# q and k loaded in 48 rows a group, and the first chunks' gates, exponents and low parts of w_in in another order

## The reference

```python
m_new = np.maximum(f_gate[:, :, t] + m, i_gate[:, :, t])
f_stab = np.exp(f_gate[:, :, t] + m - m_new)
i_stab = np.exp(i_gate[:, :, t] - m_new)
C = f_stab[..., None, None] * C + i_stab[..., None, None] * np.einsum('bhd,bhe->bhde', vt, kt)
n = f_stab[..., None] * n + i_stab[..., None] * kt
denom = np.maximum(np.abs(np.einsum('bhd,bhd->bh', n, qt)[:, :, None]), 1.0)
y[:, :, t] = sigmoid(o_gate[:, :, t]) * np.einsum('bhde,bhe->bhd', C, qt) / denom
```

## Time and profile before

| | us |
|---|---|
| median of 3 runs | 278.72 |
| lowest and highest | 278.70, 279.81 |
| the profiled execution's own time | 278.94 |
| its span | 277.1 |

### The profile page before, as it was taken

One profiled execution on the slowest core, in us unless ns is written; L12 is line 12 of the kernel. 1 busy time (PEld: TensorE's weight loads), 2 busy tenths in 40 slices (PEclk: granted clock), 3 DMA queues, 4 the chain that ended last, 5 costly groups with the idle time before them and its releaser, 6 DMA issues.

```text
span 277.1 us, 5247 instructions
## 1 busy us (share of the span) xinstructions
PE 269.2 (97%) x1959; PEld 257.6 (93%) x1959; DVE 202.4 (73%) x367; ACT 165.7 (60%) x329; POOL 69.0 (25%) x101
## 2 busy tenths in 40 slices
PE   8889999999999999999999999999999999999995
PEld 6777989889999999999999999999999999999995
DVE  5687987787988988655467686456867776876694
ACT  7968877996886664323243212256576567666763
POOL 6484532166454322063000790000000000000000
PEclk9999999999999999999999999999999999999999
DMA  6789975465546000009400000000000000300004
GB/s 176 227 229 285 296 231 196 143 207 160 184 117 228 2 0 2 0 0 269 151 0 2 0 0 2 0 0 0 4 0 2 0 0 2 142 0 4 0 0 146
DMA packets 13258, 23.61 MB, mean 85 GB/s; under 512 B 1968, under 2 KB 7920, under 8 KB 13232
## 3 DMA queue, kind: packets, MB, share of 16 engines
q1 hardware_dynamic: 12832, 22.89, 27.1%
q10 hardware_dynamic: 400, 0.38, 0.4%
HBM read 21.25 MB, written 2.02 MB: 84 GB/s over the span
## 4 chain that ended last, share of the span: by engine, by line
PE 83%; DVE 7%; ACT 6%; issue 2%; DMA 1%; SPq 0%; DVEq 0%; ACTq 0%
PE bank L592 18%; PE bank L649 14%; PE bank L634 14%; PE bank L617 8%; PE bank L578 7%; PE bank L559 7%; PE bank L536 6%; PE bank L506 3%; PE bank L514 2%; PE bank L542 1%; DMA og_b<-og 1%; PE bank L525 1%; DVE win_lo L988 1%; ACT decay L751 1%; DVE decay L983 1%
## 5 line engine op out<-in xcount | busy, mean ns | idle before, releaser
L592 PE MATMUL bank<-wsp_hi,vn_hi 128*128 128x384 f32 x96 | 32.2, 335 | 0.0
L592 PE MATMUL bank<-wsp_lo,vn_hi 128*128 128x384 f32 x96 | 32.1, 334 | 0.0
L592 PE MATMUL bank<-wsp_hi,vn_lo 128*128 128x384 f32 x96 | 32.1, 334 | 0.0
L796 ACT ACTIVATE gt_hi<-gated_t 128x384 fp32r<-128x384 f32 x16 | 8.4, 524 | 37.1 <-DVE gated_t L1117 37.1
L649 PE MATMUL bank<-wo_hi,hg_hi 128*128 128x320 f32 x96 | 29.8, 311 | 0.3 <-DVE hg_lo L1167 0.3
L649 PE MATMUL bank<-wo_lo,hg_hi 128*128 128x320 f32 x96 | 29.6, 308 | 0.0
L649 PE MATMUL bank<-wo_hi,hg_lo 128*128 128x320 f32 x96 | 29.6, 308 | 0.0
L1150 DVE SCALAR_TENSOR_TENSOR tap<-h,conv_w,tap 128x768 f32<-128x768 f32 (+1 forms) x17 | 16.5, 970 | 17.5 <-ACT tap L828 17.5
L751 ACT ACTIVATE decay<-log_in,cols 128x128 f32<-128x128 f32 x80 | 25.5, 391 | 4.1 <-PE bank L536 4.0
L536 PEld LDWEIGHTS bank<-v_aug,decay 128*128 128x128 f32 x192 | 24.0, 191 | 2.6 <-DVE decay L983 1.3
L834 ACT ACTIVATE gate<-convd 128x768 f32<-128x768 f32 (+1 forms) x17 | 13.8, 809 | 19.3 <-DVE convd L1154 19.3
(11 more groups left out here) (171 smaller groups left out, 766.7 us busy)
## 6 DMA issues: line engine op xcount, KB each, us to landing
qk<-qk SPq DMA_DIRECT2D x24, 160.0 KB
log_in<-neg_m SPq DMA_DIRECT2D x10, 256.0 KB, 5.0
wsp_raw<-w_sp SPq DMA_DIRECT2D x6, 384.0 KB, 3.9
win_raw<-w_in SPq DMA_DIRECT2D x4, 512.0 KB, 5.6
v_aug<-v SPq DMA_DIRECT2D x12, 168.0 KB, 4.4
kw<-k SPq DMA_DIRECT2D x10, 160.0 KB, 4.9
out<-y SPq DMA_DIRECT2D x10, 160.0 KB, 1.9
og_b<-og SPq DMA_DIRECT2D x3, 480.0 KB, 9.9
```

The source lines that it names most:

```text
L592: op = pe.matmul(p_mix[m % 2][:, 0:NB], vs[:, b * NC + c, ds_], ws[:, c, ts], start=(i == 0), stop=(i == len(terms) - 1))
```

## The change

Seven things are altered, all of them before about chunk 3 except the first, which holds for every chunk.

1. q and k come in pieces of 48 rows a group in place of 40. The array in DRAM has the eight further rows, which hold zeros.
2. On SP, one load of og is left ahead of q and k (chunk 0's); og of chunks 1 and 2 is one load behind chunk 1's v. v of chunk 0 goes ahead of the second piece of chunk 0's q and k.
3. On ACT only chunk 0's gates are opened first. Chunks 1 and 2 are opened together in step n = 1, behind `xt_high(0)`, with a change of table to Sigmoid and one back. The memset of `win5_lo` goes from ACT to DVE.
4. On ACT both groups' exponents of chunk 0 come ahead of the gates' exponents (`gate_g`, `gate_w`), and `pad_log(2)` behind these. On DVE `weigh(0, 0)` comes ahead of `gate_diag`. On PE `first_logs(1, 0)` comes ahead of `columns()`.
5. The v half of w_in is split by its two blocks of 128 rows: ACT makes two high parts, DVE makes the first low part ahead of `combine(0)` and the second behind `xt_low(0)`. In every `hidden_v` the product with the second low part is the last one, and in chunk 0 it has a wait of its own.
6. `narrow_copy` of the v half goes behind the exponents of chunk 1.
7. `to_state(2)` moves from the end of step 1 into step 2, behind `in_chunk(2, 0)`, and `new_state(2)` on DVE behind `weigh(2, 1)`.

```diff
@@ SP
-            for g, ps in enumerate((rows(0), rows(1))):
+            for g in range(G):
                 if n == 0 and g:
                     load_k(0)
+                    load_v(0)
                     sp.wait_ge(sem("pad0_high"), 1)
-                sp.dma_start(qk_in[n % RING][ps, :, :, :].rearrange("p a j t -> p (a j t)"), qk[n, ps, :]
+                sp.dma_start(qk_in[n % RING][g * LO:g * LO + QR, :, :, :].rearrange("p a j t -> p (a j t)"),
+                             qk[n, g * QR:(g + 1) * QR, :]
                              ).then_inc(sem(f"ld_qk{n % RING}"), 16)
...
-        for c in range(3):
-            sp.dma_start(og_b0[:, c, :], og[:, c, :]).then_inc(sem(f"ld_og{c}"), 16)
+        sp.dma_start(og_b0[:, 0, :], og[:, 0, :]).then_inc(sem("ld_og"), 16)
         load_qk(0)
         load_in(v_half, "v")
-        load_v(0)
...
         load_v(1)
+        sp.dma_start(og_b0[:, 1:3, :], og[:, 1:3, :]).then_inc(sem("ld_o0a"), 16)
@@ PE, hidden_v
+            last = products.pop()
+            products += [(xt5[p][:, cs], win5_hi[:, fs]), (xt5[p][:, cs], win5_lo[:, fs]), last]
             for i, (lhs, rhs) in enumerate(products):
+                if n == 0 and i == len(products) - 1:
+                    pe.wait_ge(sem("win_low"), 2)
@@ PE, the order
         scores(0)
-        columns()
         pe.wait_ge(sem("neg_ready"), 1)
         first_logs(1, 0)
+        columns()
...
             in_chunk(n, 0)
+            if n == 2:
+                to_state(n)
             hidden_v(n - 1)
...
-            if gives_state(n + 1):
+            if gives_state(n + 1) and n > 1:
                 to_state(n + 1)
@@ ACT
-        for c in range(3):
-            act.wait_ge(sem(f"ld_og{c}"), 16)
-            act.activation(o_gate(c), o_gate(c), ACT.Sigmoid).then_inc(sem("o_ready"), 1)
-            if c == 0:
-                pad_log(2)
+        open_gates(0)
...
         exp_log(0, 0)
+        exp_log(0, 1)
         act.wait_ge(sem("logs_ready"), 2)
         act.activation(sc["g"][:, :], sc["glog"][:, :], ACT.Exp).then_inc(sem("gw_ready"), 1)
         act.activation(sc["w"][:, :], sc["wlog"][:, :], ACT.Exp).then_inc(sem("gw_ready"), 1)
-        exp_log(0, 1)
-        act.activation(win5_lo[LO:128, :].rearrange("p (x t) -> p x t", x=8),
-                       ident[LO:128, :].unsqueeze(1).to_broadcast([LO, 8, 128]), ACT.Copy, scale=0.0).then_inc(sem("win_ready"), 1)
+        pad_log(2)
         narrow_high("v", v_half)
-        win_high("v", v_half)
-        pad_log(0)
+        for t in range(2):
+            win_high("v", v_half, slice(t, t + 1))
         exp_log(1, 0)
-        narrow_copy("v", v_half)
+        pad_log(0)
...
             if n == 1:
+                narrow_copy("v", v_half)
                 xt_high(0)
+                open_gates(1)
@@ DVE
         dve.tensor_copy(cols[:, 2, :], p_cols[:, 2, 0:R]).then_inc(sem("cols_ready"), 1)
+        dve.memset(win5_lo[LO:128, :].bitcast(F32), 0.0).then_inc(sem("win_ready"), 1)
...
+        weigh(0, 0)
         dve.wait_ge(sem("gw_ready"), 1)
         dve.tensor_scalar(diag_dec[:, :], ident[0:R, 0:R], sc["g"][:, L - 1:L], None, ALU.mult
                           ).then_inc(sem("diag_ready"), 1)
-        weigh(0, 0)
         weigh(0, 1)
...
-        first_low(0, v_half)
+        first_low(0, v_half, slice(0, 1))
...
             weigh(n, 0)
-            if n == 2:
-                new_state(n)
             xt_low(n - 1)
+            if n == 1:
+                first_low(1, v_half, slice(1, 2))
...
             weigh(n, 1)
-            if n == 1:
+            if n in (1, 2):
                 new_state(n)
```

More of the change, by code:

```diff
@@ L22 @@
 KS = LO + D
+QR = 48
 EARLY = 2
@@ L549, in hidden_v @@
                 pe.wait_ge(sem("win_ready"), 1)
-                pe.wait_ge(sem("win_hi"), 3)
+                pe.wait_ge(sem("win_hi"), 4)
                 pe.wait_ge(sem("win5_low"), 1)
@@ L565, in hidden_u @@
             if gr == 0 and pair == 0:
-                pe.wait_ge(sem("win_hi"), 6)
+                pe.wait_ge(sem("win_hi"), 7)
                 pe.wait_ge(sem("win5_low"), 2)
-                pe.wait_ge(sem("win_low"), 2)
+                pe.wait_ge(sem("win_low"), 3)
                 pe.wait_ge(sem("exp_done"), 2 * EARLY)
@@ L715, in open_gates @@
         def open_gates(i):
-            act.wait_ge(sem(("", "ld_o0b", "ld_o1", "ld_o1")[i]), (0, 16, 32, 32)[i])
-            piece = og_b0[:, 3:6, :] if i == 1 else og_b1[i - 2][:, :, :]
+            act.wait_ge(sem(("ld_og", "ld_o0a", "ld_o0b", "ld_o1", "ld_o1")[i]), (16, 16, 16, 32, 32)[i])
+            piece = (og_b0[:, 0:1, :], og_b0[:, 1:3, :], og_b0[:, 3:6, :], og_b1[0], og_b1[1])[i][:, :, :]
             act.activation(piece, piece, ACT.Sigmoid).then_inc(sem("o_ready"), 1)
@@ L850, in write_y, with win_high @@
                     act.dma_start(out[b, c * L:(c + 1) * L, :], y[:, c, :]).then_inc(sem("stored"), 16)
-        def win_high(half, cs):
+        def win_high(half, cs, ts):
             act.wait_ge(sem(f"ld_win{half}"), 16)
-            act.activation(win_hi[:, :, cs], win_raw[:, :, cs], ACT.Copy).then_inc(sem("win_hi"), 1)
+            act.activation(win_hi[:, ts, cs], win_raw[:, ts, cs], ACT.Copy).then_inc(sem("win_hi"), 1)
         def narrow_high(half, cs):
@@ L860, in narrow_copy @@
         def narrow_copy(half, cs):
-            act.wait_ge(sem("win_hi"), 1 if half == "v" else 5)
+            act.wait_ge(sem("win_hi"), 1 if half == "v" else 6)
             act.activation(win5_hi[LO:128, cs], win5_hi[0:K5, cs].bitcast(F32), ACT.Copy).then_inc(sem("win_hi"), 1)
         exp_log(0, 0)
+        exp_log(0, 1)
         act.wait_ge(sem("logs_ready"), 2)
@@ L892, in scalar_program @@
             if n == 2:
-                open_gates(1)
+                open_gates(2)
             if n > 2:
@@ L898, in scalar_program @@
             if n == LATE:
-                open_gates(2)
                 open_gates(3)
+                open_gates(4)
             if n + 1 < NS:
@@ L984, in weigh, with first_low @@
                               ).then_inc(sem("weights_ready"), 1)
-        def first_low(i, cs):
-            dve.wait_ge(sem("win_hi"), (2, 4)[i])
-            dve.tensor_tensor(win_lo[:, :, cs], win_raw[:, :, cs], win_hi[:, :, cs].bitcast(F32), ALU.subtract
+        def first_low(i, cs, ts):
+            dve.wait_ge(sem("win_hi"), (2, 3, 5)[i])
+            dve.tensor_tensor(win_lo[:, ts, cs], win_raw[:, ts, cs], win_hi[:, ts, cs].bitcast(F32), ALU.subtract
                               ).then_inc(sem("win_low"), 1)
@@ L1075, in combine @@
             dve.wait_ge(sem("ratio_done"), n + 1)
-            if n < 3 or n % 3 == 0:
-                dve.wait_ge(sem("o_ready"), n + 1 if n < 3 else n // 3 + 3)
+            if n == 1 or n % 3 == 0:
+                dve.wait_ge(sem("o_ready"), n // 3 + 2 if n else 1)
             wait(dve, sem("xt_raw"), n)
@@ L1303, in paired @@
         a = a.reshape(B, J, G, NC, L, D).transpose(0, 3, 2, 5, 1, 4).reshape(NS, G, D, J * L)
-        t = np.zeros((NS, KS, J * L), np.float32)
-        t[:, 0:D], t[:, LO:KS] = a[:, 0], a[:, 1]
+        t = np.zeros((NS, G * QR, J * L), np.float32)
+        t[:, 0:D], t[:, QR:QR + D] = a[:, 0], a[:, 1]
         return t
```

9 lines of the change are left out of this document (4 added, 5 removed).

## The result

The changed kernel is slower: 280.86 us (median of 18 executions, 279.47 to 281.57) against 279.06 (18 executions) for the kernel before, a ratio of 1.0049, 95% [1.0032, 1.0066]. The forecast was 278.3 us and no change that can be told; the time lies outside the forecast's range as well. In all that follows, an execution over 1.5% above the fastest of its kernel counts in the medians, but not in the ratios. The profiled execution of after took 281.11 us, its span 279.3, so 2.2 us more than before.

A forecast was written before the change was run, and what follows sets the result against it. PE, busy 269.2 of 277.1 us, was taken as the bound, with DVE and ACT nearly full too at 25 to 35 us; 0.45 us gained from 278.94 gave 278.5, a median of 278.3, range 277.1 to 279.4.

The forecast's parts named there:

- The sum: Whole kernel: lead at x(0) 1.6, less 0.9 on ACT, less 0.66 on DVE, plus 0.4 of the stall: 0.45 us gained.
- The bound: PE busy 269.2 of 277.1 us; the end moves by what the start of `in_chunk(3, 0)`, 35.23, moves.
- Scores of chunk 0 at 8.1: Head: q and k land for PE's first scores at 8.1 in place of 8.68 us, floor 7.95.
- the 8% of bytes: Loads up to chunk 0's scores: 88 of 1056 KB less, worth 0.4 to 0.7 us if only bytes count.
- T = 16.45: End of `xt_high(0)` on ACT: 16.45 in place of 18.04, 1.6 us earlier; bounds 15.9 and 17.0.
- ACT carries 9.15 us: ACT from the end of `xt_high(0)` to that of `xt_high(1)`: 9.15 us back to back, with two table loads and a Sigmoid.
- So `xt_high(1)` ends ... of 1.6 us of lead 0.7 is left.: ACT in step 1: `xt_high(1)` ends at 25.6, DVE's `xt_low(1)` starts 25.65 instead of 26.36.
- Rival B: ACT's pair of table loads in step 1 becomes the bound and the kernel is slower: middle 279.4 us, chance 0.14.
- Rival D: The skill page's drain holds at ACT's table switches: 2.8 us more on ACT, 281.0 us, chance 0.02.
- `new_state(2)` ahead of `win_lo`, 0.66: DVE: `new_state(2)` now stands between `weigh(2, 1)` and `win_lo`, costing 0.66 us of lead.
- The stall of `shift`, 0.4: DVE at 32.77: `shift` took 1.10 us beside POOL's mask; an earlier mask gains 0.4 us, bounds 0.95 gained, 0.7 lost.
- The other chunks' 48 rows add 64 KB each to queues that have room after 35 us ..., and PE waits for none of them.: DMA queues of later chunks: 0.63 busy after 35 us, so the added rows cost nothing.

The follow-up runs named there:

- e1: The changed kernel again, word for word: 280.98 us, ratio 1.0048 to the kernel before.
- e7: The changed kernel with the gates of chunks 3 to 5 opened one step later (n = 3): 280.38 us, ratio 1.0048.
- e11: The changed kernel with 40 rows and `to_state(2)`, `new_state(2)` where they stood before: 280.89 us, ratio 1.0058.
- e8: The kernel before with only the new order of the head (parts 4, 5, 6, memset on DVE), 40 rows, three gates first: 279.01 us, ratio 0.9989.
- e12: e8 with two matmuls of no use in PE's gap of 0.51 us ahead of `hidden_v(1)`: 279.10 us, ratio 1.0002.
- e3: The kernel before with q and k loaded in 48 rows a group, nothing else: 280.70 us, ratio 1.0038.
- e14: e8 with one single-element Sigmoid behind `xt_high(0)`, which brings two table loads in step 1: 279.30 us, ratio 0.9995.
- e9: e8 with `to_state(2)` and `new_state(2)` moved as in the change: 279.05 us, ratio 0.9992.
- e5: The kernel before again, word for word: 279.04 us, ratio 0.9987.
- e10: e8 with q and k in 48 rows a group as the only other edit: 280.31 us, ratio 1.0032.
- e2: The changed kernel with q and k loaded in 40 rows a group again: 280.46 us, ratio 1.0054.
- e4: The changed kernel with the gates of chunks 0 to 2 loaded and opened first again: 283.22 us, ratio 1.0104.
- e6: The changed kernel with three matmuls of no use in PE's gap ahead of `hidden_v(1)`: 280.32 us, ratio 1.0043.
- e13: e11 with four matmuls of no use in PE's gap ahead of `hidden_v(1)`: 279.77 us, ratio 1.0020.

## Why the prediction was wrong, point by point

The sum gave a gain of 0.45 us where 1.8 us were lost. Two of its steps failed: ACT's lateness was priced only as a later start of DVE's chain, and the other chunks' 48 rows were put at nothing. The rest of the list says what each term measured.

- **The bound.** Right: PE is busy almost throughout, and the stretch to 35 us decides. After it the kernel runs nearly as a block: the shift is 1.85 us at `in_chunk(3, 0)` and 2.2 at the end of the span.
- **Scores of chunk 0 at 8.1.** In the changed kernel they never came so early: 9.01, 8.91 and 8.73 us in after, e1 and e7, with PE slow ahead of them. The wait itself did go: in none of the seven profiles with one load of gates ahead does PE wait for q and k. 8.1 was reached in e11 (8.17) and e8 (8.18), both released by `gate_wlog`. But e8 has 40 rows and the loads in the order of before, with no byte fewer ahead, and e12, with the same loads, waited until 8.87. So the landing moves by over 0.6 us between executions of like loads, and the 8% of bytes can't be read out of single profiles. The step's aside on the Trainium skill (DMA: Bandwidth & Descriptors, "Why a DMA increments its semaphore by 16 and not by 1"), that 48 rows go over more engines than 40, is not borne out as a gain: the 48 rows took more engine time and in e3 the first scores waited 0.98 us.
- **T = 16.45.** Mis-sized: 17.84 in the profiled execution, 16.82 in e1, 17.10 in e8. The lead was 0.2, 1.2 and 0.9 us, not 1.6. I gave no place to PE's slow head (1.65 us for six log matmuls instead of 0.99), which the trace of before didn't show; the wait that would have hidden it was the one removed.
- **ACT carries 9.15 us.** Right to 0.03 us (9.12 in after and in e1). No drain shows: the next instruction starts within 0.02 us of a table load's end. The Trainium skill (ScalarE: Activation LUTs, "What ACT_TABLE_LOAD costs") would add a drain of 1.38 us to each switch, and the trace disagrees.
- **"So `xt_high(1)` ends ... of 1.6 us of lead 0.7 is left."** This is the first step that failed. I priced ACT's lateness only as a later start of DVE. It also lengthens PE's idle gap ahead of `hidden_v(1)`, because PE kept its lead: 0.51 before, 0.88, 0.89 and 1.32 in after, e1 and e11. Behind it the granted clock fell to its lower level, for about 3 us, in the profiles of after and e1 (in e11's it did not), and 20 of 29 executions were low, against 10 of 123 before. That is 1.41 us in the profiled execution and 1.1 us between the medians of after's low and full-clock executions. Rival B named the place and the direction ("it is slower", ACT's pair of table loads) but not the clock, and its price for T = 17.84 was 280.0; its mechanism bare, e14, costs next to nothing. Rival D's 281.0 is the number nearest to the 280.86 measured, by luck: the drain that it rests on is in no row.
- **`new_state(2)` ahead of `win_lo`, 0.66.** The order came as forecast (28.76, then `win_lo` at 29.45), but with no cost that can be told beside e8 (e9).
- **The stall of `shift`, 0.4.** It went: `shift` took 0.15 us in after. But it took 0.16 in e5 too, the kernel before run again, where `in_chunk(3, 0)` started at 34.89 instead of 35.23. So the stall belonged to one execution and not to the kernel, and the 0.4 counted chance as a gain. When the logs were late a stall came elsewhere, in `win_lo` beside POOL (e3, e10, and e2 with 40 rows); in after `win_lo` took 1.23 us.
- **"The other chunks' 48 rows add 64 KB each to queues that have room after 35 us ..., and PE waits for none of them."** This is the second step that failed. The term was 0 and measures 0.38% in the kernel before (e3) and 0.43% on the head order (e10), about 1.2 us. I looked at the share after 35 us only. From 20 to 35 us the queues were full already, the share was 1.01 in the kernel before:
```profile
20.00:35.00 15.00, 14.49 (x157) 12.71 (x155) 12.04 (x27) 13.30 (x29) 8.07 (x10) 1.00 1.01 283
```
  There the q and k of the next chunks stand ahead of logs and gates. PE indeed doesn't wait for q and k; POOL and ACT wait for what is queued behind them, and DVE's `win_lo` is the victim. The cost of the rows is shown by e3 and e10, this path only by their single profiles: a mask of chunk 3's logs after 26 us stands in four of seven profiles with 48 rows (after, e3, e4, e10; not e1, e6, e7) and in one of ten with 40 (e2).
- **Why the terms don't add up.** With the gates' cost in place, no cost of the rows on top is to be seen (e11 1.0058, e2 1.0054, after 1.0049, each to about 0.0025). My reading, not shown, is that the gap at 27 us and the late data lie beside each other, so that e2, e4, e6 and e7 each took away one of two causes and changed little. e8 with one part added each (e10, e11) shows that each part costs by itself, 0.43% and 0.69% over e8, where the whole change costs 0.60%. In the whole kernel with the gap filled (e6, 1.0043) against the same with 40 rows and old states (e13, 1.0020) the difference is 0.23%, which lies within the intervals.
- **Open.** Why an unlike share of executions drops the clock at nearly equal gaps (0.77 in e14: 2 of 12; 0.90 in e7: 3 of 11; 0.88 in after: 20 of 29) is not settled; only profiled executions show where it fell. Also open are which of Sigmoid, gate load and v's place makes e11 slower than e14, and why packets of 48 rows take more engine time.
